# K rows loaded once and their turned columns copied on chip, in a chunked attention of a three-stage kernel

## The reference, cut to what matters

```python
def _attn_ref(q, k, v, mem_k, mem_v):          # B, H, S, D = 4, 8, 768, 64; n_mem = 8
    chunk, left_ctx, right_ctx = (32, 16, 8)
    for c in range(S // chunk):
        c_start = c * chunk
        c_end = c_start + chunk
        l_start = max(0, c_start - left_ctx)
        r_end = min(S, c_end + right_ctx)
        q_c = q[:, :, c_start:c_end]
        k_full = np.concatenate([mem_k, k[:, :, l_start:r_end]], axis=2)
        v_full = np.concatenate([mem_v, v[:, :, l_start:r_end]], axis=2)
        scores = scale * np.matmul(q_c, k_full.transpose(0, 1, 3, 2))
        scores = scores - np.max(scores, axis=-1, keepdims=True)
        a = np.exp(scores)
        a = a / (np.sum(a, axis=-1, keepdims=True) + 1e-09)
        out[:, :, c_start:c_end] = np.matmul(a, v_full)

def reference(...):
    x = attn_out.transpose(0, 2, 1, 3).reshape(B * S, H * D)
    x = _moe_ref(x, phi, w1, w2)                # 8 experts x 4 slots, softmax over tokens and over slots
    return _moe2_ref(x, w_gate, w_output_gate, w1, w2)   # each token goes to one of 8 experts
```

## Time and profile before

| | |
|---|---|
| median of 3 executions | 534.45 us (530.59 to 537.67) |
| the profiled execution | 533.35 us, its span 531.6 us |
| mean granted TensorE clock | 0.950 |
| busy: PE / PEld / DVE / ACT / POOL | 466.8 / 270.1 / 211.4 / 200.1 / 132.6 us |
| moved by DMA | 97.89 MB in 122416 packets, 95680 of them under 512 B |

### The profile page before, as it was taken

How to read it: one execution, slowest core, us unless ns; L and a number is a source line. 1 busy time by engine, 2 the same in 40 slices (tenths; PEclk the granted TensorE clock), 3 DMA queues, 4 the chain that set the end, 5 groups by cost and what they waited for, 6 DMA issues and landing times.

```text
span 531.6 us, 11272 instructions
## 1 busy us (share of the span) xinstructions
PE 466.8 (88%) x3674; PEld 270.1 (51%) x3675; DVE 211.4 (40%) x968; ACT 200.1 (38%) x770; POOL 132.6 (25%) x125
## 2 busy tenths in 40 slices
PE   3698988988987699566869999999999999999992
PEld 3587777777775433143534444444444444444441
DVE  3677877877877351019321122212212211221210
ACT  1799998998998210011011212112111121121210
POOL 2233443433434020001301212223222212212210
PEclk9999999999999879877679999999999999999998
DMA  9999999999999999999999764011011101100000
GB/s 146 181 191 192 240 258 214 223 268 232 228 272 280 342 325 348 374 408 401 403 392 390 282 221 171 21 42 42 22 42 42 39 23 42 41 23 3 1 1 0
DMA packets 122416, 97.89 MB, mean 184 GB/s; under 512 B 95680, under 2 KB 96176, under 8 KB 122384
## 3 DMA queue, kind: packets, MB, share of 16 engines
q1 hardware_dynamic: 115072, 75.61, 52.4%
q10 hardware_dynamic: 3696, 14.68, 7.8%
q0 software_dynamic: 3616, 7.20, 4.2%
HBM read 90.78 MB, written 8.52 MB: 187 GB/s over the span
## 4 chain that ended last, share of the span: by engine, by line
PE 75%; DVE 10%; DMA 7%; issue 3%; ACT 2%; another core or an unknown queue 0%; SPq 0%; POOL 0%; ACTq 0%; DVEq 0%; POOLq 0%
PE bank L789 41%; PE bank L535 7%; DMA arena<-in_moe_w_dram 6%; PE bank L604 5%; PE bank L773 4%; DVE arena L865 4%; PE bank L550 3%; PE bank L734 2%; PE bank L580 2%; PE bank L560 2%; PE bank L614 2%; PE bank L563 1%; PE bank L574 1%; PE bank L657 1%; DVE shared L874 1%
## 5 line engine op out<-in xcount | busy, mean ns | idle before, releaser
L789 PE MATMUL bank<-arena 128*128 x496 | 225.7, 602 | 0.0
L789 PEld LDWEIGHTS bank<-arena 128*128 128x128 f32 x496 | 90.1, 191 | 103.4 <-issue 99.9
L462 POOL TENSOR_TENSOR arena<-arena,row_inv 96x1024 f32<-96x1024 f32 x32 | 60.7, 1896 | 108.3 <-DVE row_inv L858 108.3
L1041 DVE TENSOR_SCALAR arena<-bank 128x256 f32<-128x256 f32 x124 | 43.9, 417 | 99.7 <-PE bank L773 75.5
L503 POOL DMA_INDIRECT out_dram<-arena,tok_sorted x31 | 31.5, 1015 | 191.7 <-ACT arena L1170 191.7
L1170 ACT ACTIVATE arena<-bank,gate_sorted 128x512 f32<-128x512 f32 x31 | 21.3, 687 | 103.6 <-PE bank L789 103.6
L865 DVE CUSTOM_DVE_ANT_0 arena<-bank,masks 96x128 f32<-96x128 f32 x256 | 55.0, 277 | 4.3 <-PE bank L535 4.3
L1071 ACT ACTIVATE arena<-arena,neg_max 96x128 f32<-96x128 f32 x128 | 50.0, 398 | 2.2 <-issue 1.5
L1080 ACT ACTIVATE arena<-arena,neg_max 96x128 f32<-96x128 f32 x128 | 49.8, 395 | 0.0
L535 PE MATMUL bank<-arena 64*96 64x128 f32 x512 | 37.6, 287 | 10.9 <-issue 5.6
L1163 ACT COPY arena<-bank 128x128 f32<-128x128 f32 x31 | 8.2, 266 | 101.7 <-PE bank L764 101.7
(11 more groups left out here) (168 smaller groups left out, 487.4 us busy)
## 6 DMA issues: line engine op xcount, KB each, us to landing
arena<-in_moe_w_dram SPq DMA_DIRECT2D x25, 2048.0 KB, 10.5
arena<-in_moe_w_dram ACTq DMA_DIRECT2D x7, 2048.0 KB, 10.1
arena<-in_k_dram SPq DMA_DIRECT2D x32, 240.0 KB
arena<-in_v_dram SPq DMA_DIRECT2D x32, 240.0 KB
arena<-in_q_dram SPq DMA_DIRECT2D x32, 192.0 KB
arena<-in_mem_k_dram SPq DMA_DIRECT2D x32, 16.0 KB
arena<-in_mem_v_dram SPq DMA_DIRECT2D x32, 16.0 KB
arena<-rows_scratch,tok_sorted POOLq DMA_INDIRECT x31, 2.5
```

What stands on the lines that cost most here:

```text
L462: g.tensor_tensor(probs[:, t % 4], probs[:, t % 4], row_inv[:, t % 2, :].unsqueeze(2).to_broadcast([TQ, H, NK]), ALU.mult).then_inc(p_norm ...
L789: ins = mm(bank[4 + par][:, :], h_t[:, par, f * 128:(f + 1) * 128], w2_all[:, bass.ds(e * SEG + f * DM, DM)], start=(f == 0), stop=(f == K ...
L1041: ins = vec.tensor_scalar(h_t[:, j % 2, 2 * r * 128:(2 * r + 2) * 128], bank[r][:, 0:256], 0.0, None, ALU.max)
```

## The change

K: each tile loads only the rows of its window that the tile before in the batch has not loaded: 120, 80, 96, 96, 96, 96, 96 and 88 rows for the eight tiles of a batch, instead of 120 each. They are turned alone; in front of them in `k_t` stand the 0, 40, 24, 24, 24, 24, 24 and 32 columns that the window shares with the last tile's, copied from the other place of `k_t`. The eight memory rows of K are loaded and turned for the first two tiles of a batch (one for each place of `k_t`), and their columns stay there for the others. The memory rows of V are loaded for the first four tiles of a batch, one for each place of the V ring. The counts on which TensorE waits follow. The V windows and Q are loaded as before.

```diff
+        def k_rows(t):
+            ends = [min(max(TQ * i - LEFT, 0), S - CTX) + CTX for i in range(TPB)]
+            first = ends[t % TPB - 1] if t % TPB else 0
+            return first, ends[t % TPB] - first
...
             def load_kq(b, t):
                 r = t % KQV
-                start = min(max(TQ * t - LEFT, 0), S - CTX)
+                first, rows = k_rows(t)
                 until(sp, kq_turned, b, t - KQV + 1)
                 bb = 0 if b is None else b
-                sp.dma_start(heads(k_in[0:CTX, r, :]), k_bs[bb, start:start + CTX]).then_inc(kq_in[r], 16)
-                sp.dma_start(heads(k_in[CTX:NK, r, :]), mk_bs[bb]).then_inc(kq_in[r], 16)
+                sp.dma_start(heads(k_in[0:rows, r, :]), k_bs[bb, first:first + rows]).then_inc(kq_in[r], 16)
+                if t % TPB < 2:
+                    sp.dma_start(heads(k_in[rows:rows + MEM, r, :]), mk_bs[bb]).then_inc(kq_in[r], 16)
                 sp.dma_start(heads(q_in[:, r, :]), q_bs[bb, TQ * t:TQ * t + TQ]).then_inc(kq_in[r], 16)
...
                 sp.dma_start(heads(v_in[0:CTX, r, :]), v_bs[batch, start:start + CTX]).then_inc(v_arrived[r], 16)
-                sp.dma_start(heads(v_in[CTX:NK, r, :]), mv_bs[batch]).then_inc(v_arrived[r], 16)
+                if t % TPB < KQV:
+                    sp.dma_start(heads(v_in[CTX:NK, r, :]), mv_bs[batch]).then_inc(v_arrived[r], 16)
...
-                    uses = 48 * (j // KQV + 1)
-                    pe.wait_ge(kq_in[j % KQV], uses if b is None else b * (TPB // KQV * 48) + uses)
+                    pe.wait_ge(kq_in[j % KQV], kq_landings(b, j))
                     until(pe, kt_copied, b, j)
                     until(pe, qt_copied, b, j)
+                    rows = k_rows(j)[1] + (MEM if j % TPB < 2 else 0)
                     for c in range(H // 2):
-                        nc.tensor.transpose(bank[0][:, c * NK:(c + 1) * NK],
-                                            k_in[:, j % KQV, c * 128:(c + 1) * 128], ident[:, :])
+                        nc.tensor.transpose(bank[0][:, c * NK:c * NK + rows],
+                                            k_in[0:rows, j % KQV, c * 128:(c + 1) * 128], ident[0:rows, 0:rows])
...
                     until(dve, kq_turned, b, j + 1)
                     until(dve, scored, b, j - 1)
-                    vec.tensor_copy(k_t[:, j % 2].rearrange("p c t -> p (c t)"), bank[0][:, :]).then_inc(kt_copied, 1)
+                    kept = CTX - k_rows(j)[1]
+                    rows = NK - kept if j % TPB < 2 else CTX - kept
+                    if kept:
+                        until(dve, kt_copied, b, j)
+                        vec.tensor_copy(k_t[:, j % 2, :, 0:kept], k_t[:, 1 - j % 2, :, CTX - kept:CTX])
+                    vec.tensor_copy(k_t[:, j % 2, :, kept:kept + rows],
+                                    bank[0][:, :].rearrange("p (c t) -> p c t", c=H // 2)[:, :, 0:rows]).then_inc(kt_copied, 1)
```

More of the change, by code:

```diff
@@ L309, in until, with landings, kq_landings @@
                 eng.wait_ge(s, min(count, NT))
+        def landings(b, t, each):
+            per_batch = TPB // KQV * each + 16
+            uses = t // TPB * per_batch + (t % TPB // KQV + 1) * each + 16
+            return uses if b is None else b * per_batch + uses
+        def k_rows(t):
+            ends = [min(max(TQ * i - LEFT, 0), S - CTX) + CTX for i in range(TPB)]
+            first = ends[t % TPB - 1] if t % TPB else 0
+            return first, ends[t % TPB] - first
+        def kq_landings(b, t):
+            both = 48 if t % KQV < 2 else 32
+            per_batch = both + 32 * (TPB // KQV - 1)
+            uses = t // TPB * per_batch + both + t % TPB // KQV * 32
+            return uses if b is None else b * per_batch + uses
         def g_bank(e):
@@ L593, in step @@
                 if live(b, j - 4):
-                    uses = 32 * ((j - 4) // KQV + 1)
-                    pe.wait_ge(v_arrived[(j - 4) % KQV], uses if b is None else b * (TPB // KQV * 32) + uses)
+                    pe.wait_ge(v_arrived[(j - 4) % KQV], landings(b, j - 4, 16))
                     until(pe, pt_copied_dve, b, j - 3)
```

## The result

The changed kernel takes 535.62 us (median of 20, 532.82 to 539.35) where the kernel before, run in turn with it, takes 535.24 (20, 530.59 to 539.9). The ratio is 1.004, with an interval of 1.0021 to 1.0058, so it is some 2 us slower (1.1 to 3.1). That ratio leaves out executions in a second, slower state that either kernel sometimes shows, so it does not follow from the two medians, which lie only 0.4 us apart. The forecast was 533.2 us, 0.65 us faster and hidden almost wholly.

What follows compares the result with a forecast made beforehand. The prediction took the attention's chain of waits among TensorE, ScalarE and VectorE as the bound, not transfers. Turning -0.85 and copies +0.2 gave -0.65 us on a median of 533.9, so 533.2 us, range 528 to 537.5.

Steps and rivals of the forecast that it cites:

- Transfers are not waited for: Attention loads: 9.7% fewer packets release nobody sooner, as no wait stands on a landing; 0 us.
- The rival that the transfers pace the attention: Attention: DMA sets the pace, so fewer packets save 8.5 us, giving 524.7 us; chance 0.11.
- the gain that the prediction worked out by the Trainium skill's rule on the spread over engines: Attention, if transfers pace it: busiest engines carry 17% fewer packets, gain stops at some 9.8 us, giving 523.4 us.
- The copies: K^T in two VectorE copies: 0 in the loop; +0.07 us per tile in three filling tiles, +0.2 us, at most +0.7.
- block by GpSimd: New copy within SBUF beside GpSimd: costs nothing where it stands, up to the GpSimd operation's length if it came earlier.
- The turning in the step with the logits: Loop: narrower K turning saves 0.11 us in each of six steps with logits, 0.66 us, at the least 0.
- The 0.2 us allowed at the lower clock: Filling: one step more at a lower clock likely has K's turning on the path, saving 0.2 us.
- Clock: Rival on TensorE's granted clock: 0.11 us less work of 5 us per step; the loop should hold 1.00; no chance given.

Runs made afterwards that it cites:

- after_again2: The changed kernel profiled once more with nothing altered, a third look; its last scores start at 163.88 us.
- before_again1: The kernel before profiled once more with nothing altered, a second look; its last scores start at 161.72 us.
- late_start: The changed kernel with batch 0 loaded, turned and copied as before the change, the other three batches as changed; ratio 0.9987 to the kernel before.
- width_only: The kernel before with K turned over 96 rows for every tile but the first, loads and copies as before; ratio 1.0025.
- width_again: Second profile of the kernel before with only K's turning narrowed to 96 rows, first tile excepted; last scores start at 164.16 us.
- copy_only: The kernel before with one more VectorE copy of 96 elements within SBUF ahead of each K^T copy; ratio 1.0036.
- fill_cols: The changed kernel with one more 128x128 identity turned on TensorE for each of tiles 1 to 4; ratio 0.9993 to the kernel before.
- the warmed pair: The kernel before and the changed kernel, each with extra identities turned on TensorE in the filling; ratios 0.9933 and 0.9956 to the kernel before.
- warm_glue: The kernel before with identities turned in the filling, plus five ahead of each of four short TensorE waits behind the attention; ratio 0.9969.

## Why the prediction was wrong

*Transfers are not waited for.* Right. 9.7% fewer packets, a DMA share of 0.99 instead of 1.10, and from tile 4's scores to the last it takes 133.98 us instead of 133.83. The rival that the transfers pace the attention is gone, and with it the gain that the prediction worked out by the Trainium skill's rule on the spread over engines (DMA: Bandwidth & Descriptors, section "Why a DMA increments its semaphore by 16 and not by 1").

*The copies.* Right: 0.20 us for the one, 0.55 for the other, hidden in the loop by 0.5 us. In the filling the forecast was +0.07 a tile, and in two tiles that were slow in both kernels it was 4.69 and 4.72 us from scores to scores against 4.70. No block by GpSimd shows: the longest of the 28 copies took 0.245 us, has 160 columns instead of 96, and ran before GpSimd's first operation of the attention. The Trainium skill's rule on the shared port pair (SBUF — State Buffer, "Who interferes with whom") is hardly tested here: two of the 28 copies ran before that first operation and 25 start 0.12 us or more behind the one ahead of them. The copy at 23.94 us starts, by the records, 0.05 us before the end of one, and took 0.20 us like the others.

*The turning in the step with the logits.* The mechanism was read rightly and the term was mis-sized, twice. The six steps turn tiles 8, 12, 16, 20, 24 and 28. Three of these (8, 16, 24) are the first of a batch, which the change leaves at 128 rows: they still take 0.60 us in the timeline, and nothing could be saved there. And I set the 0.11 us against a start of the logits that I took from the chain. By the timeline 0.19 us lay between the end of ScalarE's copy and the logits, of which 0.14 stay. So in the steps of tiles 20 and 28 some 0.04 came (4.77 against 4.81), in that of tile 12 nothing that stands out of 4.77 to 4.92 us in either kernel: 0.1 us or so in all instead of 0.66. The 0.2 us allowed at the lower clock did not come either, as the scores of the filling wait for VectorE and not for TensorE.

*Clock.* This is the step that failed. The sum has the filling at -0.2 for the turning and +0.2 for the copies, and the clock at nothing. Measured, the attention ended 2.25 us later on average, 1.85 of it lost by tile 4's scores and the rest in the clock's second fall in `after_again2`. The rival was put as a matter of the loop, "TensorE does 0.11 us less of 5 us per step, so the loop [...] should hold it". The loop did hold it, at 1.00. I knew of four waits for K^T in the filling, and wrote that the granted clock fell there by the earlier trace rows, whose digits are all 9 at that place and show no fall; the low stretch at the start is in no record of the clock, and the one that is (0.70 from 25 to 30 us) is too short for that row. So I took the moment of the change from one level to the other as given. It isn't. It differs between executions, and the runs speak for its depending on how TensorE is occupied before it.

In the filling TensorE isn't the bound, so 0.2 us less work per tile gives 0.2 us more idle time and no earlier scores. A tile on the lower level costs 0.9 us: from tile 1's scores to tile 2's 4.70 us on the lower level and 3.80 on the higher (`before_again1`), from tile 2's to tile 3's 4.91 and 4.01. From tile 3's to tile 4's, where the V product comes in, it is 6.0 to 6.4 us on the lower level, 5.0 to 5.2 where the clock had risen early and fell again, and 4.45 where it stayed up. So an early rise gives back 0.6 us of what it gained, and the dearest is to be still low at tile 3, 1.6 us against a clock that stays up. The Trainium skill (TensorE: Matmul & The Clock Gate, section "What's actually happening") says that the array's clock is gated between two levels by how busy the engine has been; the scores of 2.02 and 1.12 us agree.

How far the runs bear this out: the last scores start at 161.23 to 162.50 us in the four profiles with the old filling (`late_start` among them), and at 162.72 to 164.82 in the six with the narrower turning (the changed kernel and `width_only`, `width_again`), without overlap. Beyond tile 4 the kernels are alike but for the one fall of `after_again2`. With the clock made equal, the attention ends at the same time (last scores at 159.50 and 159.55, one profile each).

What stays open is what in the change holds the clock low, the narrower turning or the longer wait: `copy_only`, with a longer wait alone, and `fill_cols`, with the work put back, went both ways, and a single profile is worth little where one kernel's own differ by two tiles. Also the size: the attention explains 2.25 us in the profiles, and the timings gave 2.1 and 0.9 us. Behind the last scores it takes 368.4 to 375.7 us to the end. The three profiles of the kernel before (369.3, 369.5 and 371.7) lie under or level with the four of the changed one (371.4 to 375.5), but in the warmed pair it is the other way round (375.7 without the change, 369.5 with it). Over the nine profiles with the changed loads and the eight with the old ones (`warm_glue` left out) the mean is 372.0 and 371.2 us, which is within that scatter. Whether the change costs anything there isn't settled.

## What to carry to other kernels

Work taken from an engine that waits anyway is idle time added, and on TensorE idle time may have a price of its own, in the places where the clock is still on its lower level: read those stretches by the durations of like instructions before costing an edit at nothing. Turning an identity while TensorE waits at the start gave 0.7% in one kernel and 0.4% in the other (3.6 and 2.4 us by the timings, both against the kernel before, whose attention ended 2.2 us later in the profiles), and 9.7% fewer packets in the attention gave nothing. Where a step's gain is read against the wait that is next, the time from that wait's end to the start of the instruction behind it (here 0.14 us) belongs to the sum, and the start is read from the timeline, as the chain cuts instructions that overlap. And count a saving over the steps that have it: here three of six did not.

## What the runs showed of the hardware

The granted clock in the windows does not show the first low stretch. In the changed kernel it reads 1.00 where the scores take 2.02 us:

```profile
15.00:20.00 5.00, 3.75 (x26) 3.19 (x28) 2.63 (x20) 3.98 (x20) 0.00 (x0) 1.00 0.97 150
20.00:25.00 5.00, 3.59 (x28) 3.01 (x28) 2.83 (x21) 3.71 (x18) 1.89 (x1) 1.00 0.72 138
```

So in these profiles the stretch before the clock's first fall on record has to be read from durations. An early first rise did not last: in all six profiles with fast scores from tile 1 or 2, the granted clock went back to 0.50 between 23 and 26 us. Also, an issue of 64 packets of memory rows could hold SP's queue for 3.06 us before the change; without most of them the same queue stands 41 us for permission (21.3 + 19.6), and nobody gains by it.
